# Inverse row sums by way of a DRAM row instead of TensorE transposes, in a float32 attention and two-layer kernel

## The chip, the cores and the metric

The kernel runs on one core of a Trainium2 chip. The metric is the device time of one execution in microseconds. Engines are named TensorE (PE in the profile, PEld for its weight loads), VectorE (DVE), ScalarE (ACT), GpSimd (POOL) and the sync queue (SP), which issues every DMA of this kernel. Each of them runs its instructions in program order and waits on semaphores.

## The reference

Batch 4, 8 heads, 576 positions, head dimension 64; then 2304 tokens of 512, a layer of 2048 and back.

```python
q_rot, k_rot = (rotate(q), rotate(k))
scores = scale * np.matmul(q_rot, k_rot.transpose(0, 1, 3, 2))
scores = scores - np.max(scores, axis=-1, keepdims=True)
attn = np.exp(scores)
attn = attn / (np.sum(attn, axis=-1, keepdims=True) + 1e-09)
o = np.matmul(attn, v)                    # per head, then heads side by side
x = o.transpose(0, 2, 1, 3).reshape(B * S, H * D)
h = x @ w_in
g = np.maximum(h, 0.0) + alpha * np.minimum(h, 0.0)
out = g @ w_out
```

## The kernel before

**Precision.** Every product is made of float32r parts: an operand is split into `hi` (a rounded copy, by ScalarE) and `lo` (the rest, by VectorE subtracting), and the products hi x hi, hi x lo, lo x hi are summed.

**Periods and slots.** Attention works on pairs of heads, 16 periods (4 batches of 4 pairs), and a 17th, shorter one that finishes the last pair. In period p TensorE makes the scores of pair p, turns (transposes) its exponentials, multiplies the turned exponentials of pair p-1 with V, and turns rotated Q and K of pair p+1. The 576 rows of two heads are 9 score tiles: tile 0 holds the 64 remaining rows of both heads, tiles 1 to 4 are head 0, tiles 5 to 8 head 1. A period has 9 slots, one for each tile. In a slot each engine has a fixed order: TensorE score, then the slot's units, then one part of the value product (`PV_IN`, slots 0 to 7; in slot 0 the product comes ahead of the units); ScalarE the hi copies of the slot's units, then the exponential with its row sum (`exps`), then, in every second slot, `minor` (half of an output tile is brought to the other half of the partitions); VectorE the row maximum (`maxima`), `total` (adds the other half into `y`), steps of the reciprocal, and the lo parts of the units.

**Units.** Each unit is one fill of a PSUM bank with up to four transposes. Units are numbered in the order in which they are issued, and alternate between two banks `t_ps[u % 2]`. A unit's fill waits until the one before the last was evacuated: TensorE, ScalarE's hi, VectorE's lo, then TensorE again. `UNITS_IN` says which units stand in which slot. U_KREM and U_PB belong to head 1 of the running pair's predecessor, U_Q, U_K and U_QKREM to the next pair, U_PA, U_QREM and U_KQREM to the current one. A hi copy of U_PA waits until head 0's value products of this period are done (`pv_done` at p*4 - 2), and that of U_QREM until all of them are (`pv_done` at p*4), since the tiles they write are read by them. The last value product of a period is in slot 7. Exponential 0 of the next period waits until KQREM was turned; the score of tile n waits for the exponential of tile n-2.

**Row sums.** The exponentials leave the row sums of a pair in `rsum` [128 rows, 9 tiles]. The value product comes out with features on partitions and rows along the free axis, so the inverse sums must lie along the free axis too, repeated over 64 partitions for each head. Before the change: VectorE adds 1e-9 in slot 1, takes the reciprocal in slot 2, spreads it to `inv_wide` (128x512) in slot 3; TensorE turns that in four transposes (U_INV) and the remaining rows in a fifth (U_INV_REM) in slot 4; ScalarE copies both from PSUM to `inv_sb` [128, 576]. GpSimd's `normalise` multiplies `y` with `inv_sb` into `x` near the end of the period.

**GpSimd** in each period: the rotation of the next pair's K (`rope`, four operations; its first two wait for the raw K load), the two halves of the V split for head 0, Q's rotation for the pair after (its third operation waits until U_QKREM was turned), V's split for head 1, `normalise`.

**The sync queue** in each period: raw K for p+1 and raw Q for p+2, V, then the stacking of Q (six copies between partitions, which wait for U_Q) and of K (four copies, which wait for U_QKREM); K stacked is needed by score 1 of the next period. In periods 0 to 2 a 1 MB slice of `w_in` follows, the last slice in period 15. After the periods it issues eight loads of `w_out`, the first as soon as the last U_PB was turned.

**The layer** works in six chunks of 384 tokens and 16 blocks of 128 features. For block f TensorE makes `hidden(f)` and then `output(f-1)`; ScalarE makes the positive part and g_hi, VectorE the gate, GpSimd g_lo. In the first chunk VectorE also splits `w_in` and `w_out` into hi and lo, block by block; blocks 0 and 1 of `hidden` already run inside the 17th period. In the last batch VectorE splits a quarter of the first chunk's x at the end of slot 4.

Of the kernel before, what the change touches and what calls it, by code (L numbers as in the profile page):

```python
# [12 lines left out]
P = 128  # L13
# [13 lines left out]
TILES = 9  # L27
# [9 lines left out]
U_INV, U_INV_REM = 6, 7  # L37
U_Q, U_K, U_QKREM = 5, 8, 11
U_PA = (9, 10, 12, 13)
U_QREM, U_KQREM = 14, 15  # L40
UNITS = 16
OF_PREV = (U_KREM, *U_PB, U_INV, U_INV_REM)
# [3 lines left out]
UNITS_IN = ((0, 1), (2,), (3, 4), (5,), (6, 7), (8, 9), (10, 11), (12, 13), (14, 15))  # L46
HIDDEN_IN = (0, 2)
PV_IN = tuple((head, h, part) for head in range(2) for h in range(2) for part in range(2))


def build(nc, q, k, v, w_in, w_out, alpha, cos, sin, eye, out):
# [18 lines left out]
    PADDED = 13  # L70
# [35 lines left out]
    def hi_count(p, u):  # L106

        return tally(p, u, [w for w in range(UNITS) if w not in (U_INV, U_INV_REM)])

# [10 lines left out]
    v_h = v.rearrange("b h s d -> (b h) s d")  # L120

    with ExitStack() as ctx:
# [24 lines left out]
        with ExitStack() as att:  # L147
            rot_q = sb(att, "rot_q", [P, ST, P])
            rot_k = sb(att, "rot_k", [P, ST, P])
            cos_sb = sb(att, "cos_sb", [P, ST, D])  # L150
            sin_sb = sb(att, "sin_sb", [P, ST, D])
            q_hi = sb(att, "q_hi", [P, QT * P], F32R)
            q_lo = sb(att, "q_lo", [P, QT * P], F32R)

            k_hi = [sb(att, f"k_hi{i}", [P, REM + S], F32R) for i in range(2)]
            k_lo = [sb(att, f"k_lo{i}", [P, REM + S], F32R) for i in range(2)]


            q_two = [sb(att, "q_two0", [P, 2, QT * P], F32R)]

            q_own = [sb(att, f"q_own{i}", [P, 2, QT * P], F32R) for i in range(2)]
            assert used[0] >= 4 * CT * F
            raw_v = sb(att, "raw_v", [P, ST, P])
            qrem_hi = sb(att, "qrem_hi", [P, P], F32R)
            qrem_lo = sb(att, "qrem_lo", [P, P], F32R)


            prob = sb(att, "prob", [P, QT, 2 * S])
            prob_rem = sb(att, "prob_rem", [P, S + REM])

            pt_hi = sb(att, "pt_hi", [P, 2 * QT + 1, S], F32R)
            pt_lo = sb(att, "pt_lo", [P, 2 * QT + 1, S], F32R)

            v_a = sb(att, "v_a", [P, ST, P], F32R)
            v_b = sb(att, "v_b", [P, ST, P], F32R)
            y = sb(att, "y", [P, S])
            inv_sb = sb(att, "inv_sb", [P, S])
            nmax = sb(att, "nmax", [P, 2, TILES])
            rsum = sb(att, "rsum", [P, 2, TILES])
            inv = sb(att, "inv", [P, 2, TILES])  # L180
            inv_wide = sb(att, "inv_wide", [P, QT, P])
            ident = sb(att, "ident", [P, P])
            zero = sb(att, "zero", [P, 1])
            kept = used[0]
            q_two.append(sb(att, "q_two1", [P, 2, QT * P], F32R))
            k_two = [sb(att, f"k_two{i}", [P, 2, REM + S], F32R) for i in range(2)]
# [48 lines left out]
        wide_done = sem("wide_done")  # L235
# [44 lines left out]
        def _(sp):  # L280
# [40 lines left out]

            sp.dma_start(sin_sb[:, :, :], sin).then_inc(sin_in, 16)
# [11 lines left out]
            def batch(b):  # L334
                for t in range(PAIRS):
# [5 lines left out]
                    load_v(b, t)  # L341
                    if has_pair(p + 1):
                        stack(p + 1, (t + 1) % 2, 0)
                        stack(p + 1, (t + 1) % 2, 1)
# [8 lines left out]

# [23 lines left out]
        def _(pool):  # L377
# [38 lines left out]

            def normalise(b, t):
# [3 lines left out]
                pool.wait_ge(evac[U_INV_REM % 2], evac_count(p + 1, U_INV_REM))  # L421
# [18 lines left out]
            def batch(b):  # L440
                for t in range(PAIRS):
                    p = b * PAIRS + t
                    if has_pair(p + 1):
                        rope(p + 1, 1)
                    split_v(p, 0)
# [16 lines left out]

            low(0, 0, 0)
# [10 lines left out]
        def _(pe):  # L474
# [52 lines left out]
            def turn(p, t, u):  # L527
# [18 lines left out]
                elif u == U_INV:  # L546
                    pe.wait_ge(wide_done, p)
                    blocks = [inv_wide[:, i, :] for i in range(QT)]
                else:
                    blocks = [inv[:, (t - 1) % 2, 0:1].to_broadcast([P, P])]  # L550
# [69 lines left out]
            def output(i, c, f):  # L620
# [7 lines left out]
                if f == 0:  # L628
                    if is_first(i, c):
                        for u in (U_INV, U_INV_REM):  # L630
                            pe.wait_ge(evac[u % 2], evac_count(PERIODS, u))
# [42 lines left out]
        def _(act):  # L674
# [52 lines left out]
            def twice(p):  # L727

                act.wait_ge(exp_done, p * TILES + 1)
                nc.scalar.activation(prob_rem[:, S:S + REM], prob_rem[:, QT * P:S], ACT.Copy).then_inc(twice_done, 1)  # L730

# [10 lines left out]
            def inverse(p, u):  # L742

                act.wait_ge(turned, unit_count(p, u))
                if u == U_INV and not (isinstance(p, int) and p == 1):
                    act.wait_ge(x_done, p - 1)
                bank = t_ps[u % 2]
                if u == U_INV:
                    ins = nc.scalar.activation(inv_sb[:, 0:QT * P], bank, ACT.Copy)
                else:  # L750
                    for r in HEADS:
                        ins = nc.scalar.activation(inv_sb[r, QT * P:S], bank[r, r], ACT.Copy)
                ins.then_inc(evac[u % 2], 1)

            def period(b, t):

                p = b * PAIRS + t
                for slot in range(TILES):
                    for u in UNITS_IN[slot]:
                        if exists_now(p, u):  # L760
                            inverse(p, u) if u in (U_INV, U_INV_REM) else hi(p, u, t)
# [4 lines left out]
                    if slot == 4 and has_now(p):  # L766
                        twice(p)
# [61 lines left out]
        def _(dve):  # L829
# [8 lines left out]
            def lo(p, u, t):  # L838

                dve.wait_ge(hi_done, hi_count(p, u))  # L840
# [30 lines left out]
            def reciprocals(p, t, step):  # L871

                par = (t - 1) % 2
                if step == 0:
                    dve.wait_ge(exp_done, p * TILES)
                    nc.vector.tensor_scalar(rsum[:, par, :], rsum[:, par, :], 1e-9, None,
                                            ALU.add).then_inc(sum_done, 1)
                elif step == 1:
                    dve.wait_ge(sum_done, p)
                    nc.vector.reciprocal(inv[:, par, :], rsum[:, par, :]).then_inc(inv_done, 1)  # L880
                else:
                    dve.wait_ge(inv_done, p)
                    if not (isinstance(p, int) and p == 1):
                        dve.wait_ge(turned, unit_count(p - 1, U_INV))
                    nc.vector.tensor_copy(inv_wide[:, :, :].rearrange("p i (h d) -> p i h d", h=2),
                                          inv[:, par, 1:].rearrange("p (h i) -> p i h", h=2)
                                          .unsqueeze(3).to_broadcast([P, QT, 2, D])).then_inc(wide_done, 1)
# [54 lines left out]
            def period(b, t):  # L942

                p = b * PAIRS + t
                for slot in range(TILES):
# [7 lines left out]
                    if 1 <= slot <= 3 and has_prev(p):  # L953
                        reciprocals(p, t, slot - 1)
                    if not has_now(p) and slot < len(HIDDEN_IN):
                        split_w_in(slot)
                    for u in UNITS_IN[slot]:
                        if exists_now(p, u) and u not in (U_INV, U_INV_REM):
# [7 lines left out]
            nc.vector.memset(zero[:, :], 0.0).then_inc(padded, 1)  # L966

# [70 lines left out]
```

## Time and profile before

| | us |
|---|---|
| median of three timed runs | 758.29 |
| lowest and highest of them | 755.85, 759.17 |
| the profiled execution | 754.38 |
| its span, first to last instruction | 752.6 |
| TensorE busy in the span | 698.5 |
| VectorE busy | 468.9 |
| ScalarE busy | 384.7 |
| GpSimd busy | 324.5 |

The profile comes from one execution, which was a little quicker than the timed ones. The granted TensorE clock was 0.999 over the span. Attention takes up the first 331 us or so; there the three busy engines are all far more occupied than their share of the whole span says.

### The profile page before, as it was taken

Reading aid. Unit: us, or ns where it says so; the run is one execution under the profiler, and the core shown is the slowest. Engines: PE = TensorE matmul, PEld = TensorE weight load, DVE = VectorE, ACT = ScalarE, POOL = GpSimd, SP = SyncE. Lnnn points to the kernel's source line nnn. Section 1 sums busy time; section 2 is a strip of 40 time slices with the busy share of each in tenths; the row PEclk is TensorE's granted clock in tenths of the full one; section 3 lists DMA queues with packets and bytes.
Section 4 is the critical chain, followed back from the end, with each engine's and each line's share of the span. In section 5 each row is a group of like instructions: output and inputs, shape, how many; then the busy total and the mean of one; then the engine's idle time right before and its main releaser. Section 6 shows DMA issues by size and latency. Waiting matters only on the chain.

```text
span 752.6 us, 12908 instructions
## 1 busy us (share of the span) xinstructions
PE 698.5 (93%) x4164; PEld 630.8 (84%) x4164; DVE 468.9 (62%) x841; ACT 384.7 (51%) x900; POOL 324.5 (43%) x312
## 2 busy tenths in 40 slices
PE   4888999999999999887999999999999999999996
PEld 3777888888888888877988999999999999999995
DVE  4798888888888999978998324333323332332321
ACT  2788888888888888863222322222232222223222
POOL 6477777777777777212322222222222222222221
PEclk9999999999999999999999999999999999999999
DMA  7766745555555454506000100000010001000001
GB/s 163 187 162 130 170 113 115 118 121 124 124 124 119 109 114 102 147 8 217 1 0 1 43 1 2 14 29 1 0 42 0 0 0 42 0 0 29 15 1 42
DMA packets 76621, 51.32 MB, mean 68 GB/s; under 512 B 61088, under 2 KB 61472, under 8 KB 76064
## 3 DMA queue, kind: packets, MB, share of 16 engines
q1 hardware_dynamic: 76576, 50.76, 27.1%
q8 instruction: 24, 0.39, 0.2%
q14 instruction: 21, 0.17, 0.1%
HBM read 22.95 MB, written 4.72 MB: 37 GB/s over the span
## 4 chain that ended last, share of the span: by engine, by line
PE 49%; issue 19%; DVE 13%; ACT 9%; POOL 4%; DMA 2%; SPq 2%; POOLq 0%; ACTq 0%; DVEq 0%
PE banks L615 17%; PE banks L643 16%; PE banks L552 8%; DVE pt_lo L865 5%; PE banks L579 4%; ACT prob L690 3%; PE banks L523 3%; ACT pt_hi L724 3%; DVE nmax L835 2%; POOL g_lo L460 2%; DMA raw_k<-in_k 1%; DVE y L894 1%; PE banks L492 1%; SPq L306 1%; DVE w_out_hi L925 1%
## 5 line engine op out<-in xcount | busy, mean ns | idle before, releaser
L460 POOL TENSOR_TENSOR g_lo<-g,g_hi 128x384 fp32r<-128x384 f32 x96 | 102.3, 1066 | 309.6 <-ACT g_hi L788 309.6
L936 DVE TENSOR_SCALAR g<-banks,alpha_sb 128x384 f32<-128x384 f32 x96 | 59.3, 618 | 223.4 <-ACT pos L780 223.2
L780 ACT ACTIVATE pos<-banks 128x384 f32<-128x384 f32 x96 | 47.1, 491 | 167.6 <-PE banks L615 167.5
L615 PE MATMUL banks<-x_hi,w_in_hi 128*128 128x384 f32 x384 | 129.9, 338 | 0.5 <-issue 0.5
L615 PE MATMUL banks<-x_lo,w_in_hi 128*128 128x384 f32 x384 | 129.4, 337 | 0.0
L615 PE MATMUL banks<-x_hi,w_in_lo 128*128 128x384 f32 x384 | 129.2, 336 | 0.0
L865 DVE TENSOR_TENSOR pt_lo<-banks,pt_hi 128x512 fp32r<-128x512 f32 x192 | 112.2, 607 | 14.7 <-ACT pt_hi L724 11.3
L643 PE MATMUL banks<-w_out_hi,g_hi 128*128 128x512 f32 x288 | 113.5, 394 | 7.2 <-DVE y L894 3.0
L788 ACT ACTIVATE g_hi<-g 128x384 fp32r<-128x384 f32 x96 | 50.4, 525 | 129.6 <-DVE g L939 129.6
L835 DVE TENSOR_REDUCE nmax<-banks 128x1 f32<-128x576 f32 x144 | 108.3, 752 | 13.3 <-PE banks L523 12.5
L724 ACT ACTIVATE pt_hi<-banks 128x512 fp32r<-128x512 f32 x192 | 97.6, 533 | 31.1 <-PE banks L552 28.1
L643 PE MATMUL banks<-w_out_hi,g_lo 128*128 128x512 f32 x288 | 113.0, 392 | 0.0
L643 PE MATMUL banks<-w_out_lo,g_hi 128*128 128x512 f32 x288 | 112.5, 391 | 0.0
L552 PE MATMUL banks<-ident,prob 128*128 128x128 f32 x576 | 85.8, 280 | 24.2 <-DVE pt_lo L865 11.8
L552 PEld LDWEIGHTS banks<-ident,prob 128*128 128x128 f32 x576 | 63.3, 141 | 42.6 <-DVE pt_lo L865 30.6
L690 ACT ACTIVATE prob<-banks,nmax 128x576 f32<-128x576 f32 x128 | 94.6, 739 | 4.2 <-DVE nmax L835 3.4
L615 PEld LDWEIGHTS banks<-x_hi,w_in_hi 128*128 128x128 f32 x384 | 72.0, 188 | 4.6 <-issue 0.7
L615 PEld LDWEIGHTS banks<-x_lo,w_in_hi 128*128 128x128 f32 x384 | 72.3, 188 | 3.6
L615 PEld LDWEIGHTS banks<-x_hi,w_in_lo 128*128 128x128 f32 x384 | 72.1, 188 | 0.0
L643 PEld LDWEIGHTS banks<-w_out_hi,g_hi 128*128 128x128 f32 x288 | 54.1, 188 | 17.2 <-issue 6.4
L643 PEld LDWEIGHTS banks<-w_out_hi,g_lo 128*128 128x128 f32 x288 | 54.1, 188 | 12.1
L643 PEld LDWEIGHTS banks<-w_out_lo,g_hi 128*128 128x128 f32 x288 | 54.2, 188 | 8.4
(97 smaller groups left out, 1207.2 us busy)
## 6 DMA issues: line engine op xcount, KB each, us to landing
k_two<-k_hi SPq DMA_DIRECT2D x64, 160.0 KB, 2.8
out<-stage SPq DMA_DIRECT2D x18, 256.0 KB, 2.0
raw_q<-in_q SPq DMA_DIRECT2D x32, 128.0 KB, 2.5
raw_k<-in_k SPq DMA_DIRECT2D x32, 128.0 KB, 2.7
q_two<-q_hi SPq DMA_DIRECT2D x32, 128.0 KB, 2.4
q_two<-q_lo SPq DMA_DIRECT2D x32, 128.0 KB, 2.4
q_own<-q_hi SPq DMA_DIRECT2D x32, 128.0 KB, 2.4
raw_v<-in_v SPq DMA_DIRECT2D x32, 128.0 KB, 2.3
```

Source lines behind the costliest of these rows:

```text
L460: nc.gpsimd.tensor_tensor(g_lo[f % 2][:, :], g[f % 2][:, :], g_hi[f % 2][:, :].bitcast(F32), ALU.subtract).then_inc(g_lo_done, 1)
L552: mm = nc.tensor.transpose(bank[:, i * P:(i + 1) * P], block_in, ident[:, :])
L579: mm = nc.tensor.matmul(o_ps[h], vv[:, j, :], pt[:, slot, cols], start=(j == 0 and k == 0), stop=(j == QT and k == 1))
L615: mm = nc.tensor.matmul(h_ps[f % 2], w[:, j, cols], xx[:, j, :], start=(step == 0), stop=(step == 3 * CT - 1))
L643: mm = nc.tensor.matmul(y_ps[c % 2][m], lhs[j][f % 2][:, m * P:(m + 1) * P], rhs[j][:, f, :], start=(f == 0 and j == 0), stop=(f == FT - 1 ...
L690: nc.scalar.activation(dst.rearrange("p (h s) -> p h s", h=2), s_ps[(t * TILES + n) % 2], ACT.Exp, bias=nmax[:, t % 2, n:n + 1], accum_out ...
L724: ins = nc.scalar.activation(dst, src, ACT.Copy, scale=scale)
L780: nc.scalar.activation(pos[f % 2][:, :], h_ps[f % 2], ACT.Relu).then_inc(pos_done, 1)
L788: nc.scalar.activation(g_hi[f % 2][:, :], g[f % 2][:, :], ACT.Copy).then_inc(g_hi_done, 1)
L835: nc.vector.tensor_reduce(nmax[:, t % 2, n:n + 1], s_ps[(t * TILES + n) % 2], AX.XY, ALU.max, negate=True).then_inc(max_done, 1)
L865: ins = nc.vector.tensor_tensor(dst, src, high.bitcast(F32), ALU.subtract)
L936: nc.vector.tensor_scalar(g[f % 2][:, :], h_ps[f % 2], 0.0, alpha_sb[:, f:f + 1], ALU.min, ALU.mult).then_inc(neg_done, 1)
```

## The change

The inverse sums no longer pass through TensorE. GpSimd adds 1e-9 (`guard`, at the head of its period, as an add of a 1-column tile `tiny`), VectorE takes the reciprocal in slot 3, and the sync queue stores the 9 columns into a DRAM row (`inverse_out`) and, when that has landed, loads it back with a broadcast over 64 partitions per head (`inverse_in`, four loads). The units U_INV and U_INV_REM are gone; those behind them move up by a place or so: U_K from slot 5 to 4, the second U_PA from slot 6 to 5, U_PA's third from 7 to 6, U_QREM from slot 8 to 7. ScalarE's small copy `twice` becomes an add of zero on GpSimd, behind K's rotation. `normalise` waits for the loads.

```diff
-U_INV, U_INV_REM = 6, 7
-U_Q, U_K, U_QKREM = 5, 8, 11
-U_PA = (9, 10, 12, 13)
-U_QREM, U_KQREM = 14, 15
-UNITS = 16
+U_Q, U_K, U_QKREM = 5, 6, 9
+U_PA = (7, 8, 10, 11)
+U_QREM, U_KQREM = 12, 13
+UNITS = 14
...
-UNITS_IN = ((0, 1), (2,), (3, 4), (5,), (6, 7), (8, 9), (10, 11), (12, 13), (14, 15))
+UNITS_IN = ((0, 1), (2,), (3, 4), (5,), (6,), (7, 8), (9, 10), (11, 12), (13,))
+INV_IN = 3
...
+    inv_rows = nc.dram_tensor("inv_rows", (2, TILES * P), F32, kind="Internal").ap()
...
+            def inverse_out(p, par):
+
+                sp.wait_ge(inv_done, p)
+                sp.dma_start(inv_rows[par].rearrange("(n p) -> p n", p=P), inv[:, par, :],
+                             allow_slow_non_contiguous=True).then_inc(inv_out, 16)
+
+            def inverse_in(p, par):
+
+                sp.wait_ge(inv_out, p * 16)
+                for h in range(2):
+                    for to, first in ((slice(0, QT * P), P + h * QT * P), (slice(QT * P, S), h * REM)):
+                        count = to.stop - to.start
+                        sp.dma_start(inv_sb[h * D:(h + 1) * D, to],
+                                     inv_rows[par:par + 1, first:first + count].to_broadcast([D, count])
+                                     ).then_inc(inv_in, 16)
...
                     load_v(b, t)
+                    if has_prev(p):
+                        inverse_out(p, (t - 1) % 2)
                     if has_pair(p + 1):
                         stack(p + 1, (t + 1) % 2, 0)
+                    if has_prev(p):
+                        inverse_in(p, (t - 1) % 2)
+                    if has_pair(p + 1):
                         stack(p + 1, (t + 1) % 2, 1)
...
             batches(sp, batch)
-
+            inverse_out(PERIODS, 1)
+            inverse_in(PERIODS, 1)
...
+            def guard(p, par):
+
+                pool.wait_ge(exp_done, p * TILES)
+                nc.gpsimd.tensor_tensor(rsum[:, par, :], rsum[:, par, :], tiny[:, :].to_broadcast([P, TILES]),
+                                        ALU.add).then_inc(sum_done, 1)
+
+            def twice(p):
+
+                pool.wait_ge(exp_done, p * TILES + 1)
+                nc.gpsimd.tensor_tensor(prob_rem[:, S:S + REM], prob_rem[:, QT * P:S],
+                                        zero[:, :].to_broadcast([P, REM]), ALU.add).then_inc(twice_done, 1)
...
-                pool.wait_ge(evac[U_INV_REM % 2], evac_count(p + 1, U_INV_REM))
+                pool.wait_ge(inv_in, (p + 1) * 64)
...
+                    if has_prev(p):
+                        guard(p, (t - 1) % 2)
                     if has_pair(p + 1):
                         rope(p + 1, 1)
+                    twice(p)
                     split_v(p, 0)
...
+            guard(PERIODS, 1)
             low(0, 0, 0)
...
-            def inverse(p, u):
...
-                    if slot == 4 and has_now(p):
-                        twice(p)
...
-                    if 1 <= slot <= 3 and has_prev(p):
-                        reciprocals(p, t, slot - 1)
+                    if slot == INV_IN and has_prev(p):
+                        reciprocals(p, (t - 1) % 2)
```

## Rows read from the trace of the kernel before

**Rows 1.** The page's first line.

```profile
span 752.6 us, 12908 instructions
```

**Rows 2.** Busy time by stretch: an attention period, and eight us of the layer.

```profile
core 0: us, PE busy (x) PEld busy (x) DVE busy (x) ACT busy (x) POOL busy (x), PEclk, DMA share, GB/s
200.66:220.24 19.58, 17.97 (x136) 16.41 (x135) 17.58 (x34) 17.22 (x44) 14.12 (x14) 1.00 0.52 119
...
353.00:361.00 8.00, 8.00 (x42) 7.33 (x41) 7.79 (x12) 1.94 (x4) 2.60 (x2) 1.00 0.00 0
```

**Rows 3.** The chain that ended last, 218.5 to 232.5: start, duration, what.

```profile
220.10 0.56 PE banks L552 x5
...
221.62 0.84 ACT prob L690 x2
...
222.50 0.66 PE banks L552 x4
223.16 0.79 PE banks L579 x6
223.95 0.55 PE banks L523 x4
...
230.63 0.84 ACT prob L690 x2
...
231.61 0.65 PE banks L552 x4
```

**Rows 4.** ScalarE's instructions in order of time, slots 7 and 8.

```profile
229.25 0.40 ACT L739 ACTIVATE y<-banks 64x288 f32<-64x288 f32 x1
229.68 0.93 ACT L724 ACTIVATE pt_hi<-banks 128x512 fp32r<-128x512 f32 x3
```

**Rows 5.** Single lines' instructions: duration in ns (min/median/max), first and last start.

```profile
L876 DVE TENSOR_SCALAR rsum<-rsum x16: 161/321/832, 36.1 to 333.2; 128x9 f32<-128x9 f32 x16
...
L885 DVE COPY inv_wide<-inv x16: 410/419/1632, 40.0 to 338.2; 128x512 f32<-128x512 f32 x16
...
L730 ACT ACTIVATE prob_rem<-prob_rem x16: 243/244/245, 24.5 to 321.4; 128x64 f32<-128x64 f32 x16
```

**Rows 6.** VectorE in order of time, slots 6 and 7 of the next period.

```profile
244.32 0.76 DVE L835 TENSOR_REDUCE nmax<-banks 128x1 f32<-128x576 f32 x1
...
246.21 0.45 DVE L867 SCALAR_TENSOR_TENSOR qrem_lo<-banks,qrem_hi 64x64 fp32r<-64x64 f32 x2
```

**Rows 7.** GpSimd and TensorE in order of time, period 2.

```profile
62.70 1.54 POOL L400 TENSOR_TENSOR rot_k<-rot_k,swapped 128x640 f32<-128x640 f32 x1
...
64.39 0.63 PE L492 MATMUL banks<-ident,rot_k 128*128 128x128 f32 x4 [1.02 <-POOL rot_k L400]
```

**Rows 8.** GpSimd in order of time, an ordinary period.

```profile
237.06 1.56 POOL L400 TENSOR_TENSOR rot_k<-rot_k,swapped 128x640 f32<-128x640 f32 x1
```

**Rows 9.** The sync queue in order of time, the same period.

```profile
240.04 0.49 SPq L305 DMA_DIRECT2D q_two<-q_hi  x1
...
246.99 0.46 SPq L305 DMA_DIRECT2D k_two<-k_hi  x1
```

**Rows 10.** DMA views, 210 to 218.5 and 220 to 226.5: packets, MB, share; issues.

```profile
q1 hardware_dynamic: 3813, 1.27, 63.8%
...
raw_v<-in_v SPq DMA_DIRECT2D x2, 16.0 KB, 2.1
...
q1 hardware_dynamic: 480, 0.79, 55.0%
```

**Rows 11.** The end of attention: sync queue, landing times, VectorE, TensorE.

```profile
336.91 8.55 SPq L361 DMA_DIRECT2D w_out_raw<-in_moe_w_out  x8
...
DMA to landing us min/median/max: 3.3/6.0/7.4
...
338.16 0.42 DVE L885 COPY inv_wide<-inv 128x512 f32<-128x512 f32 x1
...
344.08 0.43 DVE L925 CAST w_out_hi<-w_out_raw 128x512 fp32r<-128x512 f32 x1
...
346.54 0.47 PE L643 MATMUL banks<-w_out_hi,g_hi 128*128 128x512 f32 x1 [3.02 <-DVE y L894]
```

More of the change, by code:

```diff
@@ L36 @@
 U_PB = (1, 2, 3, 4)
-U_INV, U_INV_REM = 6, 7
-U_Q, U_K, U_QKREM = 5, 8, 11
-U_PA = (9, 10, 12, 13)
-U_QREM, U_KQREM = 14, 15
-UNITS = 16
-OF_PREV = (U_KREM, *U_PB, U_INV, U_INV_REM)
+U_Q, U_K, U_QKREM = 5, 6, 9
+U_PA = (7, 8, 10, 11)
+U_QREM, U_KQREM = 12, 13
+UNITS = 14
+OF_PREV = (U_KREM, *U_PB)
 OF_NEXT = (U_Q, U_K, U_QKREM)
-UNITS_IN = ((0, 1), (2,), (3, 4), (5,), (6, 7), (8, 9), (10, 11), (12, 13), (14, 15))
+UNITS_IN = ((0, 1), (2,), (3, 4), (5,), (6,), (7, 8), (9, 10), (11, 12), (13,))
 HIDDEN_IN = (0, 2)
+INV_IN = 3
 PV_IN = tuple((head, h, part) for head in range(2) for h in range(2) for part in range(2))
@@ L69, in build @@
     PERIODS = NB * PAIRS
-    PADDED = 13
+    PADDED = 14
     Q_STACKED, K_STACKED = 6 * 16, 4 * 16
@@ L104, in unit_count @@
         return tally(p, u, range(UNITS))
-    def hi_count(p, u):
-        return tally(p, u, [w for w in range(UNITS) if w not in (U_INV, U_INV_REM)])
     def evac_count(p, u):
@@ L180, in build @@
             inv = sb(att, "inv", [P, 2, TILES])
-            inv_wide = sb(att, "inv_wide", [P, QT, P])
             ident = sb(att, "ident", [P, P])
             zero = sb(att, "zero", [P, 1])
+            tiny = sb(att, "tiny", [P, 1])
             kept = used[0]
@@ L234, in build @@
         inv_done = sem("inv_done")
-        wide_done = sem("wide_done")
+        inv_out, inv_in = sem("inv_out"), sem("inv_in")
         twice_done = sem("twice_done")
@@ L545, in turn @@
                     blocks = [prob_rem[:, QT * P:S + REM]]
[L546 to L550, printed above, removed]
                 for i, block_in in enumerate(blocks):
@@ L629, in output @@
                     if is_first(i, c):
-                        for u in (U_INV, U_INV_REM):
+                        for u in U_PB[2:]:
                             pe.wait_ge(evac[u % 2], evac_count(PERIODS, u))
@@ L725, in hi @@
                 ins.then_inc(hi_done, 1)
-            def twice(p):
-                act.wait_ge(exp_done, p * TILES + 1)
-                nc.scalar.activation(prob_rem[:, S:S + REM], prob_rem[:, QT * P:S], ACT.Copy).then_inc(twice_done, 1)
             def minor(p, head, h):
@@ L740, in minor @@
                                      ACT.Copy).then_inc(minor_done, 1)
-            def inverse(p, u):
[L744 to L753, printed above, removed]
             def period(b, t):
@@ L760, in period @@
                         if exists_now(p, u):
-                            inverse(p, u) if u in (U_INV, U_INV_REM) else hi(p, u, t)
+                            hi(p, u, t)
                     if has_now(p):
@@ L838, in lo @@
             def lo(p, u, t):
-                dve.wait_ge(hi_done, hi_count(p, u))
+                dve.wait_ge(hi_done, unit_count(p, u))
                 bank = t_ps[u % 2]
@@ L869, in lo, with reciprocals @@
                 ins.then_inc(evac[u % 2], 1)
[L871 to L887, printed above, removed]
+            def reciprocals(p, par):
+                dve.wait_ge(sum_done, p)
+                nc.vector.reciprocal(inv[:, par, :], rsum[:, par, :]).then_inc(inv_done, 1)
             def total(p, head, h):
@@ L957, in period @@
                     for u in UNITS_IN[slot]:
-                        if exists_now(p, u) and u not in (U_INV, U_INV_REM):
+                        if exists_now(p, u):
                             lo(p, u, t)
@@ L966, in _ @@
             nc.vector.memset(zero[:, :], 0.0).then_inc(padded, 1)
+            nc.vector.memset(tiny[:, :], 1e-9).then_inc(padded, 1)
             dve.wait_ge(padded, PADDED)
```

## The prediction

> **What bounds the kernel now.** I read the page first: one core, a span of 752.6 us [rows 1]. The timed median is 758.29 us and the profiled execution itself took 754.38 us, so sums below are made on 754.38 and then carried over to the median as a difference. The stage table then splits the span: attention up to about 331 us, the gated layer behind it. One attention period of 19.58 us holds 17.97 us of TensorE, 17.58 of VectorE and 17.22 of ScalarE [rows 2]: three engines, each in order, each about 90% full, handing two PSUM banks round. So the length of a period is set by the chain of waits, not by any one busy sum, and an instruction counts only where the chain runs through it. In the layer TensorE is full (8.00 of 8.00 us) with VectorE at 7.79 [rows 2]; what is late at its start stays late.
>
> The chain through one period [rows 3]: TensorE reaches the five inverse-sum transposes at 220.10, after a stretch of unbroken TensorE work that began with slot 1; ScalarE evacuates them (220.66 to 221.59), does the exponential of tile 4 at 221.62, and only then may TensorE turn `prob` at 222.50. From there TensorE, and twice a bank hand-over, lead to ScalarE's run in slots 7 and 8 (exp 7, minor, three copies of units QREM and KQREM, exp 8 [rows 4]), whose end releases the next period's first transposes at 231.61. I call that instant R.
>
> **Removed and moved, step by step.**
> Slots 0 to 3: nothing on TensorE changes. VectorE loses the add on `rsum` (161 to 832 ns, median 321) and the wide copy (410 to 1632 ns) and keeps a 0.2 us reciprocal [rows 5]. From R to the inverse transposes TensorE is the chain in the period shown, so there it gives 0. In other periods the add stands between a maximum and a `pt_lo`; I take 0.2 us on average, bounds 0 and 0.4.
> Slot 4: the five transposes (0.56 us) become the four of U_K, and ScalarE's inverse copies (0.96 us from 220.66 to 221.62) become one hi copy of 0.5. Exp 4 starts at 221.19, `prob` can be turned at 222.07 instead of 222.50: gain 0.43. Four of the five transposes are thereby not saved but replaced by U_K's, which leave slot 5, where TensorE had been waiting for exp 4 anyway. The 0.24 us copy `twice` [rows 5] goes to GpSimd between the K rotation and `split_v`; before, ScalarE did it after exp 4, beside TensorE's wait. GpSimd had 5.4 us free in the period [rows 2], so it costs nothing there; without that cover it would be its own 0.3 to 0.4 us.
> Slots 5 to 8: the unit numbering shifts by one place, and this is the step that decides. Slot 5 now holds PA0 and PA1, slot 6 QKREM and PA2, slot 7 PA3 and QREM, slot 8 KQREM alone. In units of the chain (four transposes 0.54, or 0.66 after a wait; a six-matmul product 0.79; a score 0.54; a four-matmul product 0.54 [rows 3]) TensorE runs from 222.07: PA0 0.66, PA1 0.54, product 0.79, score 0.54, QKREM 0.22, PA2 0.54, product 0.54, score 0.54 = 226.44. PA3 must wait for the bank of QKREM: score 6 is done at 224.9 (0.3 behind its last issue), so VectorE's maximum (0.76 [rows 6]) ends at 225.7, the y total, which waits for ScalarE's minor copy, at 226.1, and QKREM's three small subtractions (two of them 0.45 [rows 6]) at 226.8. PA3 at 226.82, QREM behind it, product 7 until 228.81. Now ScalarE: its hi copy of QREM waits for `pv_done` of p*4, which is the product of slot 7. Before, that copy stood in slot 8, behind exp 7, and the wait was long over. Now it stands in front of exp 7. ScalarE has nothing queued ahead of it but PA3, idles about 0.8 us until 228.87, and everything behind it follows: QREM 0.5, exp 7 0.85, minor 0.43, KQREM 0.45, exp 8 0.84 and 0.14 to TensorE [rows 3, 4] = 232.08. R was 231.61. So a period gets 0.47 longer in spite of 0.43 won in slot 4. Late with it is next period's score 0 (it waits for exp 7). If no bank wait stood before PA3 and QREM, R would be 231.5, a gain of 0.1: these are the bounds. Less the 0.2 of the add I take +0.27 for each of 15 periods: +4.0 (bounds -4 and +8).
>
> Periods 1 to 3: K's rotation is late there, since the raw K load stands behind a 1 MB weight load. In period 2 it ends at 64.24 and U_K is turned at 64.39 after 1.02 us of waiting, in slot 5, with exp 4 done [rows 7]; `prob` follows at once (+0.47). In slot 4 the same wait holds the hi copy, and exp 4 stands behind that on ScalarE: `prob` comes 0.54 + 0.5 + 0.84 and the hand-overs = 1.94 after U_K. That is 1.47 later, 1.9 against an ordinary period; the K stacking and with it the raw load come some 0.7 earlier, which leaves 1.2, three times = +3.6. The copy of 1632 ns [rows 5] stood on the chain in period 1; that gives back 1.5. Together +2.1 (bounds 0 and +5). In ordinary periods the rotation ends at 238.62 [rows 8], some 1.2 us before U_K's new place, where the inverse sums were. The new guard fits into GpSimd's wait for that load. In the last batch VectorE's split of x comes between lo(K) and maximum 5: +0.8 in all (0 to 2).
>
> The DRAM row: each period adds one store of 1152 elements of 4 bytes and four broadcast loads. The store waits in the sync queue for the reciprocal, behind it are six Q stackings, the four loads and the K stacking. The reciprocal is where the wide copy was, about 239.2; Q stacking began at 240.04, K stacking at 246.99 [rows 9]. The trace has no store of this kind. Lower bound: the 16 KB load's 2.1 us, plus 72 packets an engine at 22.8 ns (63.8% of 16 engines in 8.5 us over 3813 packets) = 3.7 us. Upper: at the 119 ns of the 2 KB packets (55.0% of 6.5 us over 480) = 10.7 [rows 10]. The packets are smaller than any shown, so I take 4.5. It lands at 243.8, four issues of 0.62 end at 246.3, before K's copy is ready: hidden. Up to about 6 us it stays so (the new period also leaves K's stacking more time); beyond that each us is lost 15 times, since raw K and K's stack stand behind. Inverse rows land by 248.5, `normalise` starts at about 251: hidden.
> By the Trainium skill, "DMA: Bandwidth & Descriptors", Rules for kernel authors, a last dimension that is not contiguous becomes one descriptor per element; the same page's Specifications say that transfers under 512 B are read-modify-write. No row here shows a 4-byte write. By that rule the store would lie near the upper price of [rows 10], and the sum would be (10.7 - 6) x 15 = 70 us higher; by the packets' price of the same rows it adds nothing.
>
> The end of attention: the `w_out` loads were issued at 336.91 [rows 11]; now the sync queue first waits for the last reciprocal (338.4, where the copy was [rows 11]), the store (4.5) and four issues (2.5) = 345.4. A load alone needs at least 3.3 us [rows 11]: 348.7. VectorE took `w_out` at 344.08, and the last total, the x scaling and GpSimd's next g_lo are queued behind it; TensorE's first output product at 346.54 had all of it [rows 11]. So 348.7 - 344.1 = 4.6 late, plus 0.6 for the last `w_in` slice, whose load also moves behind a store: +5.2 (3.5 to 9). The saved inverse copies vanish in this wait. Nothing later gives it back [rows 2].
>
> Sum: 4.0 + 2.1 + 0.8 + 5.2 = +12.1, 766.5 on the profiled scale, 770 on the median's.
>
> **Rivals.** (a) Faster: the three engines lose 0.56, 1.2 and 0.8 us of work a period, and if the bank hand-overs, with two units fewer, give more than the QREM wait takes, a period could end 0.9 shorter: -13.5, +5.2 at the end, -1.5 in periods 0 and 1: 748.5. For it: twelve small idles at hand-overs; against: the chain had TensorE full from slot 1 to 4 and the wait on `pv_done`. It decides as soon as a period saves over 0.35. (b) No change: bank waits in slots 6 and 7 don't occur, periods save 0.3, the end costs 4: 757 to 760. (c) The store is slow, 8 us or more: (8 - 6) x 15 = +30 and a longer end, about 800. For it: the upper price of [rows 10]; against: its small packets are cheap. (d) The exchange by DMA saves nothing and costs nothing, only the end shows: 763, inside my range.
>
> **How the numbers follow.** Chances: my case with (d) 0.60, (b) 0.18, (a) 0.14, (c) 0.08. A measurement of this kernel tells about 0.5% (3.8 us) from no change. Faster (under 754.5) 0.14, within 0.5% 0.18, slower 0.68. The low end leaves (a) out, 754. The high end is all upper bounds without (c): 8 + 5 + 2 + 9 = +24, with a little of a slow store, 785.
>
> **What would show it.** ScalarE idle of 0.5 to 1 us before the QREM copy, released by TensorE's product, in each period; exp 7 behind it; periods of 19.7 to 20.2 us; U_K waiting over 1 us for `rot_k` in periods 1 to 3; the store 3.7 to 6 us to landing; `w_out` issued about 8.5 us after PB3 was turned, and VectorE waiting for it some 4 to 5 us. Wrong: periods under 19.3 us; no wait at QREM; K's stack late and TensorE waiting for `k_two` in slot 1 (then c).

## The result, and the profile after

The changed kernel takes 870.91 us (868.35 to 875.79 in four runs) where the kernel before takes 757.07 in the same comparison: a ratio of 1.1514, 95% interval 1.1447 to 1.1582. It is 114 us slower. I had forecast 770 us and a range from 754 to 785: the direction was right, the size far out.

The first line of the page and one line of the stretch table of the changed kernel come first; the stretch is one attention period, from one stacking of Q to the next, and answers to [rows 1, 2]. The columns are those of [rows 2].

```profile
span 870.0 us, 12725 instructions
...
231.63:258.60 26.97, 19.63 (x131) 17.82 (x130) 17.10 (x32) 16.12 (x40) 14.48 (x16) 0.87 0.85 97
```

A period is 26.97 us long instead of 19.58. TensorE has five transposes less to do and is still busy for longer, 19.63 us against 17.97, at a mean granted clock of 0.87. VectorE and ScalarE are at 17.10 and 16.12, so the removed work is gone from them. No engine is the limit. The chain of the changed kernel through the same period (compare [rows 3]) says what is:

```profile
223.35 1.33 PE banks L559 x4
224.68 0.85 PE banks L583 x4
225.54 1.44 PE banks L610 x6
...
230.64 0.13 DVE inv L885
230.77 0.02 issue
230.79 11.73 DMA inv_rows<-inv
242.51 0.03 issue
242.55 0.46 SPq L332
...
246.89 3.10 DMA k_two<-k_hi
```

The reciprocal ends, the sync queue issues the store, and the store takes 11.73 us to land. The four loads of the row wait for it and take the queue another 2.4 us; K's stacking stands behind them and lands at 250.0; only then can score 1 of the next period start, which leads to the next reciprocal. That is a closed loop of one period. Two groups of waits (who waited for whom, total, times, longest), 100 to 420 us, show where it hurts (L454 is `normalise`):

```profile
PE banks L559 <- DMA k_two<-k_hi: 59.4, 12, 6.2
POOL x L454 <- DMA inv_sb<-inv_rows: 55.4, 12, 5.9
```

The landing time is not the same in every period. The sync queue shows it as the time from the store (L323) to the first load that waits for it (L332). In ten of the fourteen periods in which Q's copies are issued behind the store it is 11.2 to 12.3 us; in the other four it is 9.3 to 9.5, as here:

```profile
285.18 0.38 SPq L323 DMA_DIRECT2D inv_rows<-inv  x1
...
294.62 2.39 SPq L332 DMA_DIRECT2D inv_sb<-inv_rows  x4
```

The two last stores, with nothing behind them, take 9.3 us each. The fifteen stores ahead of the last come to 11.1 us on average. What sets the four short ones apart is not shown.

The loop has a second price. These are TensorE's rows of the stretch table before and after the wait (the last three figures are granted clock, DMA share, GB/s):

```profile
244.00:250.00 6.00, 0.56 (x6) 0.33 (x3) 1.32 (x3) 1.81 (x4) 1.55 (x2) 0.79 0.78 189
250.00:252.00 2.00, 1.97 (x9) 1.96 (x9) 0.60 (x1) 0.00 (x0) 0.64 (x1) 0.50 0.75 169
...
256.00:258.60 2.60, 2.60 (x21) 2.37 (x20) 2.45 (x6) 2.15 (x7) 1.02 (x3) 1.00 0.00 0
```

TensorE waits 5.47 us for `k_two` in front of score 1 and comes back at a granted clock of 0.50, the lower of its two levels (1.2 of 2.4 GHz). In the chain above a score takes 1.33 us, four transposes 0.85 and a six-matmul product 1.44, where [rows 3] have 0.55, 0.56 for five transposes and 0.79. That is some 1.8 us more in a period, all of it on the loop, on top of the wait itself.

At the end of attention (compare [rows 11]) the sync queue waits for the last store, alone in the queues this time, and `w_out` is issued at 457.53. VectorE idles 12.06 us for it and, earlier, 7.43 us for the last slice of `w_in`, which had stood behind the store of period 15:

```profile
445.75 0.37 SPq L323 DMA_DIRECT2D inv_rows<-inv  x1
455.05 2.37 SPq L332 DMA_DIRECT2D inv_sb<-inv_rows  x4
457.53 5.19 SPq L381 DMA_DIRECT2D w_out_raw<-in_moe_w_out  x8
```

```profile
435.88 0.43 DVE L915 CAST w_in_hi<-w_in_raw 128x512 fp32r<-128x512 f32 x1 [7.43 <-DMA w_in_raw<-in_moe_w_in]
...
462.51 0.43 DVE L923 CAST w_out_hi<-w_out_raw 128x512 fp32r<-128x512 f32 x1 [12.06 <-DMA w_out_raw<-in_moe_w_out]
```

And ScalarE's wait at QREM, the step that the prediction called the deciding one, is there too, with 0.86 us and in the place that was named (ScalarE in order of time, slot 7; the copy of unit QREM writes `pt_hi`):

```profile
240.28 0.60 ACT L755 ACTIVATE pt_hi<-banks 128x512 fp32r<-128x512 f32 x1 [0.86 <-PE banks L610]
240.77 0.73 ACT L721 ACTIVATE prob<-banks,nmax 128x576 f32<-128x576 f32 x1
```

### The profile page after: what moved, and what is told of

Read it like the earlier page. It is cut to its first block, busy times and chain, and to the rows that moved or that the text cites. A ratio compares the mean times of both kernels' runs of the same rounds, so it can differ in the third digit from the quotient of the medians.

```text
span 870.0 us, 12725 instructions
## 1 busy us (share of the span) xinstructions
PE 724.3 (83%) x4084; PEld 656.4 (75%) x4084; DVE 459.5 (53%) x810; ACT 368.2 (42%) x836; POOL 328.4 (38%) x344
## 4 chain that ended last, share of the span: by engine, by line
PE 39%; issue 19%; DMA 18%; SPq 12%; DVE 6%; ACT 3%; POOL 2%; POOLq 0%; DVEq 0%; ACTq 0%
PE banks L646 15%; PE banks L674 14%; DMA inv_rows<-inv 11%; DMA k_two<-k_hi 5%; SPq L332 4%; PE banks L559 4%; SPq L303 3%; PE banks L583 3%; PE banks L610 3%; SPq L304 2%; POOL g_lo L495 2%; DVE pt_lo L876 2%; DVE nmax L846 1%; SPq L306 1%; ACT pt_hi L755 1%
## 5 line engine op out<-in xcount | busy, mean ns | idle before, releaser
L559 PE MATMUL banks<-k_two,q_two 128*128 128x288 f32 x252 | 63.6, 338 | 64.9 <-DMA k_two<-k_hi 64.8
L583 PE MATMUL banks<-ident,prob 128*128 128x128 f32 x576 | 93.3, 304 | 18.0 <-ACT prob L721 11.9
L559 PEld LDWEIGHTS banks<-k_two,q_two 128*128 128x128 f32 x252 | 46.5, 219 | 68.5 <-DMA k_two<-k_hi 44.4
L583 PEld LDWEIGHTS banks<-ident,prob 128*128 128x128 f32 x576 | 73.7, 156 | 32.3 <-issue 13.7
```

The source lines that it names most:

```text
L559: mm = nc.tensor.matmul(tile[:, h, :], lhs[:, :], rhs[:, first + h * HALF:first + (h + 1) * HALF], start=(j == 0), stop=(j == len(products ...
L583: mm = nc.tensor.transpose(bank[:, i * P:(i + 1) * P], block_in, ident[:, :])
```

## The experiments

Times are medians, each beside its own runs of the kernel before; those had medians of 755.1 to 755.2.

### The store taken out

```diff
-                sp.dma_start(inv_rows[par].rearrange("(n p) -> p n", p=P), inv[:, par, :], ...).then_inc(inv_out, 16)
-                sp.wait_ge(inv_out, p * 16)
-                                     inv_rows[par:par + 1, first:first + count].to_broadcast([D, count])
+                                     w_in[par:par + 1, first:first + count].to_broadcast([D, count])
```

> The changed kernel without the 1152-element store and the wait for it; the four broadcast loads read rows of w_in instead of the inverse sums (so the rows are not normalised). Everything else of the change stays: units, slots, guard and twice on GpSimd, the order of the sync queue. Theory A, the store is what costs: its 9 to 12 us stand between the reciprocal and K's stacking, 15 times, and twice more at the end; without it no wait for k_two, a granted clock of 1.0 all through, and the time that the recorded prediction gave for the rest of the change, 762 to 775 us. Rival B, the broadcast loads or the new order of the units carry a good part: still above 800 us, with waits for k_two or at the banks. Rival C, the rest of the change is a gain that the store hid: under 754 us.

The store and the wait for it are left out, and the loads read rows of `w_in` instead, so this kernel doesn't normalise. Measured: 771.34 us, ratio 1.0207 (1.0185 to 1.0229). What is left of the change costs 16.2 us, and the store with its wait is worth the other 98 of the 114 (99.6 by the two medians, but the kernel before was 2 us quicker in this comparison). Theory A holds; B and C fall. One period of this kernel:

```profile
213.38:233.40 20.02, 17.59 (x131) 15.80 (x129) 17.03 (x32) 16.18 (x40) 14.53 (x16) 1.00 0.57 131
```

20.02 us is 0.44 more than [rows 2], and the clock in this period is back at 1.00.

### The same, with QREM back behind exponential 7

```diff
-UNITS_IN = ((0, 1), (2,), (3, 4), (5,), (6,), (7, 8), (9, 10), (11, 12), (13,))
+UNITS_IN = ((0, 1), (2,), (3, 4), (5,), (6,), (7, 8), (9, 10), (11,), (12, 13))
```

> As the kernel without the store (row sums not applied, loads from w_in), with QREM moved back to slot 8 beside KQREM, slot 7 holding PA3 alone. Theory: ScalarE's hi copy of QREM waits about 0.9 us in each period for the value product of slot 7 and pushes exp 7 and exp 8; behind exp 7 it waits for nothing, and 15 periods save 0.4 to 0.5 us each: 5 to 8 us less than the kernel without the store. Rival: the bank hand-overs of slot 8 take the place of that wait, under 3 us of difference either way.

Measured: 757.47 us, ratio 1.0024 (1.001 to 1.0037), 13.9 us less than the kernel without the store. The mechanism is the one expected; the size was about double the 5 to 8 us expected. The two kernels' ScalarE waits, first over five periods with QREM in slot 7, then over six with QREM in slot 8:

```profile
ACT pt_hi L752 <- PE banks L580: 12.6, 19, 2.1
ACT pt_hi L752 <- PE banks L607: 4.3, 5, 0.9
```

```profile
ACT pt_hi L752 <- PE banks L580: 14.5, 23, 1.7
ACT q_hi L752 <- PE banks L525: 2.4, 6, 0.4
```

```profile
210.74:229.83 19.09, 17.21 (x131) 15.84 (x129) 17.03 (x32) 16.09 (x40) 14.58 (x16) 1.00 0.59 138
```

The wait for the value product (L607), 0.86 us in each period, is gone and an ordinary period is 19.09 us: 0.93 less, and 0.49 less than before the change.

### The store written as contiguous rows

```diff
-                sp.dma_start(inv_rows[par].rearrange("(n p) -> p n", p=P), inv[:, par, :],
-                             allow_slow_non_contiguous=True).then_inc(inv_out, 16)
+                sp.dma_start(inv_rows[par].rearrange("(p n) -> p n", p=P), inv[:, par, :]).then_inc(inv_out, 16)
```

> The changed kernel with the store written as 128 contiguous rows of 36 bytes instead of 1152 single elements; the loads wait for it but read rows of w_in, since the order in DRAM is another (row sums not applied). Theory A1, the number of packets is what makes the store slow: it lands in 2 to 3 us, hidden before K's stacking, and the time is that of the kernel without a store within 4 us. Rival A2, any store to DRAM with a wait on its landing in this queue costs 5 us or more: waits for k_two of some us in each period, 790 us or above.

Measured: 772.74 us, ratio 1.022 (1.0191 to 1.0248), the same as without a store. The landing time is 1.4 us (line, KB, median us to landing):

```profile
inv_rows<-inv SPq DMA_DIRECT2D x16, 4.5 KB, 1.4
```

So a store to DRAM that is waited for is harmless in this place. The same bytes written as 1152 single words side by side are not. (In this order the loads would bring the sums to the wrong places, so they read rows of `w_in` here too: this is a measurement and no repair.)

### K's stacking ahead of the loads of the row

```diff
-                    if has_prev(p):
-                        inverse_in(p, (t - 1) % 2)
                     if has_pair(p + 1):
                         stack(p + 1, (t + 1) % 2, 1)
+                    if has_prev(p):
+                        inverse_in(p, (t - 1) % 2)
```

> The changed kernel, complete, with one move in the sync queue: K's stacking is issued before the loads of the inverse sums. Theory A with the queue's order as its lever: no wait for k_two is left, but the raw K load and the loads of the inverse sums still stand behind the store; raw K comes some 4 us late, U_K in slot 4 waits some 3 us for the rotation, 15 times: about 815 us (800 to 830). If the loop through K's stacking was not what set the period, it stays at 870.

Measured: 816.52 us, ratio 1.0811 (1.0774 to 1.0847): 54 us come back by the order of the queue alone, as forecast. Its waits, 100 to 340 us:

```profile
POOL x L454 <- DMA inv_sb<-inv_rows: 52.8, 11, 6.9
...
ACT k_hi L755 <- PE banks L528: 9.7, 9, 1.9
...
PEld banks L559 <- DMA k_two<-k_hi: 9.1, 6, 2.2
```

The waits for `k_two` shrink (in the changed kernel TensorE had 46.7 us of them in the same window), though they are not gone as I had expected. GpSimd waits for the row as long as before, 4.8 us a time (4.9 in the changed kernel), but this wait now holds up the period: `normalise` starts when the row has landed, K's rotation stands behind it in GpSimd's program, and ScalarE waits for the turned K (the second line). The last two stores, alone in the queues, take 8.3 and 8.7 us, where the changed kernel has 9.3 and 9.3 for the same stores. The time was met more closely than the path: I had put it down to the raw K load.

### What makes the store slow: fewer elements, other distances, another target

All of these wait for the store and load rows of `w_in`, so the row sums are not applied. The last store is the number to read, and the one before it beside it: both are alone in the queues. Each is one store of one execution; for the same store two executions gave 8.3 to 9.3 us (above). The fourth column has all 16 stores.

```diff
-inv_rows[par].rearrange("(n p) -> p n", p=P), inv[:, par, :]
+inv_rows[par, 0:3 * P].rearrange("(n p) -> p n", p=P), inv[:, par, 0:3]      # a third
+inv_rows[par, :, 0].rearrange("(n p) -> p n", p=P), inv[:, par, :]            # inv_rows (2, TILES * P, 16), or 4, or 2
+spread[:, :, par], inv[:, par, :]                                             # spread: SBUF, [P, TILES, 2]
```

> The changed kernel storing only 3 of the 9 columns (384 elements of 4 bytes instead of 1152); the loads wait for it but read rows of w_in (row sums not applied). In the changed kernel the last store, alone in the queues, took 9.3 us to its landing: 2.1 us for a small transfer plus 6.2 ns per element. Theory A1, the time goes with the number of elements: the last store lands in 2.1 + 384 x 6.2 ns = 4.5 us, and the kernel comes within 5 us of the one without a store (771). Rival A3, a fixed delay of a store whose landing is waited for: it lands in 9 us again and the time stays above 850 us.

> The changed kernel with its 1152 elements written 64 bytes apart in DRAM instead of next to each other; the loads wait for it and read rows of w_in (row sums not applied). Rival D1, the slowness comes from neighbouring 4-byte writes meeting in one piece of memory: apart, the last store lands in under 5 us and the time falls to about 775 us. Theory D2, each 4-byte write is slow by itself: 9 us again, 865 to 880 us.

> The changed kernel with the same number of 4-byte packets, 1152, written to SBUF (every second word of a tile, same partition) instead of to DRAM; the loads wait for it and read rows of w_in (row sums not applied). If the number of packets alone is slow: last store 9 us, about 870 us. If writing small pieces to DRAM is: it lands in about 3 us and the time is 771 us within 5.

> The changed kernel with its 1152 elements 8 bytes apart in DRAM (loads from w_in, row sums not applied). Side by side the last store took 9.3 us to land, 64 bytes apart 2.8, and a third of the elements side by side still 8.1. Theory D1a, writes to one piece of 64 bytes follow each other at about 0.43 us each, and pieces run beside one another: 8 such writes to a piece, 2.4 + 8 x 0.43 = 5.8 us. Rival D1b, the whole set is serial and any distance below 64 bytes is as bad as none: above 8 us.

> The changed kernel with its 1152 elements 16 bytes apart in DRAM (loads from w_in, row sums not applied). Theory D1a: 4 writes to a piece of 64 bytes, 2.4 + 4 x 0.43 = 4.1 us for the last store. If pieces are of 32 bytes, 2 writes meet here and 4 at 8 bytes' distance: 3.2 us and 4.1. Rival D1b: above 8 us.

| store | last store to landing, us | the one before | all 16 stores | kernel, us | ratio |
|---|---|---|---|---|---|
| 1152 elements side by side (the change) | 9.3 | 9.3 | 9.3 to 12.3 | 870.91 | 1.1514 |
| 384 of them, side by side | 8.1 | 10.3 | 7.9 to 12.1 | 832.79 | 1.1026 (1.1001 to 1.1052) |
| 1152, 8 bytes apart | 5.7 | 5.1 | 4.4 to 6.4 | 780.88 | one run |
| 1152, 16 bytes apart | 3.5 | 3.6 | 3.0 to 4.8 | 776.93 | one run |
| 1152, 64 bytes apart | 2.8 | 2.9 | 2.7 to 3.4 | 775.26 | 1.0264 (1.024 to 1.0288) |
| 1152 to SBUF, 8 bytes apart | 2.4 | 2.4 | 2.4 to 3.2 | 774.55 | 1.0255 (1.0232 to 1.0279) |
| 128 rows of 36 bytes | 1.4 | 1.9 | 1.4 to 2.2 | 772.74 | 1.022 (1.0191 to 1.0248) |

The landings stand in the chains of these kernels, one line each, in the order of the table from the second row:

```profile
407.92 8.06 DMA inv_rows<-inv
```

```profile
358.24 5.74 DMA inv_rows<-inv
```

```profile
357.08 3.47 DMA inv_rows<-inv
```

```profile
355.87 2.77 DMA inv_rows<-inv
```

```profile
355.54 2.38 DMA spread<-inv
```

```profile
355.22 1.41 DMA inv_rows<-inv
```

A third of the elements still takes 8.1 and 10.3 us, so theory A1 falls: the number of elements, and with it that of packets, does not set the time. Sixty-four bytes apart the same 1152 four-byte pieces land in 2.8 us, so they are not slow by themselves either, and D2 falls. Nor is SBUF as a target slow, at 8 bytes' distance. What is slow is single words written close together in DRAM, and the closer the slower: a linear rule with 64-byte pieces (2.4 us plus 0.43 for each write that shares one, worked out from 9.3 and 2.8 us) was written down before the last two runs and gave 5.8 and 4.1 us; 5.74 and 3.47 were measured for the last store, 5.1 and 3.6 for the one before it, in one execution each. The direction is met, and the sizes within 0.7 us. The size of a piece is not settled by this. With the distance the stretch of DRAM that the store covers grows too, from 4.5 to 72 KB, and no run changes one without the other; what in the memory path makes such writes slow is open.

### The weight slices behind the raw K load

```diff
                     load_v(b, t)
+                    if isinstance(b, int) and b == 0 and t:
+                        sp.dma_start(w_in_raw[:, t - 1, :], w_in[(t - 1) * P:t * P, :]).then_inc(w_in_in, 16)
...
-                    if isinstance(b, int) and b == 0 and t < CT - 1:
-                        sp.dma_start(w_in_raw[:, t, :], w_in[t * P:(t + 1) * P, :]).then_inc(w_in_in, 16)
```

> The kernel without the store, QREM in slot 8 (757.5 us; row sums not applied), with the three 1 MB weight slices of the first periods issued one period later behind the V loads instead of between K's stacking and the raw K load. Theory: periods 1 and 2 took 25.3 and 25.9 us there against 19.1 for an ordinary one, since U_K in slot 4 stood 4 us waiting for the rotation of a late raw K; with raw K in time they fall to about 20 us and the kernel takes 745 to 749 us. Rival: the late raw K has another cause, or the slices delay Q's stacking instead: no more than 3 us of difference.

Measured: 746.72 us, ratio 0.9898 (0.9882 to 0.9915): 10.8 us less than its base. U_K in slot 4 needs the rotated K a slot earlier, and K's stacking, the weight slice and the next raw K all come after U_K: as I read the queue, a late one makes the next late. In the base kernel the waits of 42 to 93 us hold this:

```profile
POOL swapped L408 <- DMA raw_k<-in_k: 11.6, 2, 6.4
...
PE banks L525 <- POOL rot_k L417: 8.1, 3, 3.7
```

### The end of attention with the weights first

```diff
                 elif f == FT // 2:
+                    inverse_out(PERIODS, 1)
+                    inverse_in(PERIODS, 1)
                     sp.wait_ge(pv_done, 4 * PERIODS)
```

and the last `w_in` slice right behind `load_v`.

> The same base kernel (757.5 us), with only the end of the sync queue changed: the first four w_out loads and the last w_in slice are issued ahead of the last transfers of the row. Theory: w_out had been waited for 2.4 us by VectorE with the y total behind it, first output product at 351.8 against 336.2 for the last turn, 15.6 us, where the kernel before has 15.0 to 16.0 with its own work in between; what is left to win is 3 to 5 us: 752 to 755 us. Rival: the wait is hidden by the products of the last pair, no difference.

Measured: 755.10 us, ratio 1.0003 (0.9988 to 1.0019), 2.4 us less than its base, a little under the 3 to 5 that I had looked for; the intervals of the two ratios overlap, so the gain is barely clear of noise. The chain at the end shows what holds it up: the row's loads now stand behind 2 MB of weights and take 5.8 us to land, and GpSimd's x scaling, with a g_lo behind it, waits for them.

```profile
342.34 5.83 DMA inv_sb<-in_moe_w_in
```

### A complete version by way of one transpose

TensorE turns the 128x9 inverse sums in one instruction, into the free end of the bank of QKREM, VectorE copies 9x128 to SBUF, and the store has 9 rows of 512 bytes; it stands between the halves of Q's stacking. QKREM and K change places, QREM is in slot 8, and both changes of the weights' order are in.

```diff
+                nc.tensor.transpose(t_ps[U_QKREM % 2][0:TILES, BANK - P:BANK], inv[:, par, :], ident[:, :])
...
+                nc.vector.tensor_copy(row[0:TILES, :], t_ps[U_QKREM % 2][0:TILES, BANK - P:BANK]).then_inc(row_done, 1)
...
+                sp.dma_start(inv_rows[par].rearrange("(n p) -> n p", p=P), row[0:TILES, :]).then_inc(inv_out, 16)
...
+UNITS_IN = ((0, 1), (2,), (3, 4), (5,), (6,), (7, 8), (9, 10), (11,), (12, 13))
```

> A complete version, normalised rows included, that keeps the DRAM row but feeds it otherwise. TensorE turns the 128x9 inverse sums in one transpose (into the free end of QKREM's bank), VectorE copies the 9x128 row, and the store has 9 rows of 512 bytes. QKREM and K change places, QREM stands in slot 8, the weight slices go behind the V loads, and at the end the first four w_out loads go ahead of the row's transfers. Sum: 757.5 us of the kernel without a store and with QREM last, less about 10 us that periods 1 and 2 lost there to the late raw K, less 4.5 us of w_out's wait, plus 16 x 0.15 us for the turn: 743 to 750 us, faster than the kernel before. Rival: K's bank and stacking come later than QKREM's did and score 1 waits for k_two, 755 us or more.

Measured: 752.16 us (746.38 to 755.81), ratio 0.994 (0.9914 to 0.9965). It computes everything and is 0.6% faster than the kernel before; that is a smaller gain than the 743 to 750 us hoped for. In the early periods the exchange still stands in its chain:

```profile
127.70 3.46 DMA inv_rows<-row
...
133.68 0.52 SPq L307
...
137.48 2.37 DMA raw_k<-in_k
```

The store takes 3.46 us among Q's copies, the loads follow, K's stacking starts at 133.68 and raw K lands behind that. This is no longer a loop through every period: between 100 us and the end of attention the chain holds this one store alone, and an ordinary period is 19.18 us. Three of the early periods are longer (22.2, 20.1 and 21.9 us from one stacking of Q to the next), which is 6.6 us in all, by the slowest of the eight runs.

## Why the prediction was wrong

**The step that failed** is the landing time of the store: "The packets are smaller than any shown, so I take 4.5." It was 9.3 us alone and 9.3 to 12.3 with Q's copies behind it; the fifteen stores that count here took 11.1 on average. The stated bounds, 3.7 and 10.7 us, held the short ones of these and not the ten long ones. Both were worked out as so many packets by a time per packet, and the time doesn't lie in the packets: in the changed kernel the last store's 1168 packets (the DMA view of 446 to 448 us) were all on record within 1 us, and the landing was at 455.05. That the upper bound came near was luck: at 64 bytes' distance the same packets landed in 2.8 us. How close together the words lie in DRAM decides, and no row of before could show that, since none of its transfers writes single elements. With no row near it, the range should have been wider at the top and the case that hangs on it should have had more than 0.08.

**The case itself was right.** Rival (c) said: above some 6 us each us counts 15 times. With 11.1 that is 76 us, the end adds 9.3 - 4.5 = 5, and my own 12 for the rest make 757 + 93 = 850. Measured were 871. What rival (c) lacked is the clock: some 1.8 us in the period shown, at the lower level; an estimate for 15 such periods is 27 us. Together that is 6 us more than was measured. The threshold of 6 is not sharp either: with stores of 4.4 to 6.4 us (8 bytes apart, one run) the kernel was already 8 us slower than with the store of contiguous rows. The terms are not separated further by these runs.

**The rest of the sum, 12.1 us, against 16.2 measured** (771.3 without the store; it held neither the store nor its part of the end, so it is a test of the other terms). By the two traces (17.3 us apart), counted from one exponential 0 to the next, periods 1 to 3 are 6.7 us longer together, periods 7 and 8 3.1, the ten others 4.6, and what comes behind the start of period 15 2.9.
- Slots 5 to 8, +0.47 us a period from the wait of QREM's hi copy: a period went from 19.58 to 20.02 and the wait stands in the trace with 0.86 us against 0.8. Right. The forecast of the run that put QREM back was not: 13.9 us, not 5 to 8. The bank wait in front of PA3, which I had counted beside that of QREM, is the same in both kernels (TensorE 0.2 us for the lo part of K's rest, in three of three periods). What went with the wait of QREM is one of 0.8 us a period, a score that waited for an exponential.
- The 0.2 us from VectorE's add: not seen. With it a period should be 0.27 longer; the ten ordinary ones are 0.46 longer on average.
- Periods 1 to 3, +2.1: mis-sized. From the start of period 1 to that of period 4 the kernel before takes 61.6 us, 3.0 more than three ordinary periods; without the store it is 68.3, 8.2 more. So the term measured 5.2. Moving the weight slices gave back 10.8 us with QREM in slot 8, what the kernel before had lost to them included. The step was the deduction that K's stacking and raw K "come some 0.7 earlier"; U_K and everything behind it in the sync queue come later there.
- The last batch, +0.8: periods 12 to 14 together are 1.1 us longer than three ordinary ones, and were 1.0 longer in the kernel before. So this term is about 0.1.
- Not in the sum at all: periods 7 and 8 are about 2 us longer together than two ordinary ones, in the kernels without the store and not in the one before. What does it is not shown.
- The end, +5.2: in the kernel without a store VectorE waits 2.65 us for `w_out`, with it 12.06 and 7.43 more for `w_in`. The mechanism was right, and it goes by the landing time like the rest.
- Rival (a), faster: not met by the change. But the removed work is worth something. With the store, QREM's wait and the weights' order out of the way the kernel is at 746.7, 8.5 us under before; a complete version got 2.9 of that.
- Rivals (b) and (d) had the periods shorter by 0.3 or unchanged. Both are out: without the store they are longer, and with it far more so.

## What to carry to other kernels

A DMA that transposes by writing single words side by side into DRAM must not stand in a loop, and a queue in which a wait for a DMA has other work behind it makes that work part of the loop: look at what is queued behind the wait before looking at the transfer. When a unit is moved up a slot, check every wait of every engine that handles it, not only the engine from which work was removed; one such wait cost this kernel 14 us. And when no row shows a transfer of the kind that a change adds, measure it by itself first: here the bounds by packet missed most of the landings, and what sets the time was in neither.

## What the runs showed of the hardware

- 4-byte DRAM writes at 4, 8, 16 and 64 bytes' distance land in 9.3, 5.7, 3.5 and 2.8 us for the same 1152 elements. By the Trainium skill, "DMA: Bandwidth & Descriptors", Specifications, transfers under 512 B are read-modify-write. No run here shows that directly; it alone would not tell the distances apart, since at 64 bytes the pieces are as small and land in 2.8 us.
- The packet records of such a store end long before it lands: for the last one, all of them within 1 us, the landing 7 to 8 us later (446 to 448 us and 455.05 us of the changed kernel). When it is alone, DMA share and GB/s are near zero in between (the DMA view of 445.75 to 455.05 us has 5.7% in all), so these figures don't show the cost; the wait of the next instruction in the queue does.
- Transfers issued behind such a store are slowed as well, and there the profile shows it: a high DMA share with few GB/s. With Q's copies in flight the changed kernel has this (the last two figures are DMA share, which passes 1 where records overlap, and GB/s):

```profile
234.00:236.00 2.00, 2.00 (x17) 1.82 (x15) 1.21 (x3) 1.80 (x4) 0.36 (x1) 1.00 1.99 73
236.00:238.00 2.00, 1.79 (x13) 1.50 (x12) 1.91 (x7) 1.93 (x7) 1.78 (x2) 1.00 1.84 19
238.00:240.00 2.00, 1.87 (x14) 1.70 (x15) 1.88 (x4) 1.01 (x3) 1.33 (x1) 1.00 1.91 27
```

  Without the store the same copies ran at 191 and 204 GB/s and a share of 0.85 and 0.92 (171 to 175 us of that kernel). The share of a whole period rose from 0.52 to 0.85.
- TensorE, in a stretch of six us with 0.56 us of work, fell to the lower clock level; it worked at 0.50 for about four us (250 to 254) before 1.00 returned.
